# Six consecutive rows of a head per partition for q and k

## The reference

```python
q_d = q.reshape(B, H, Sd, 4, D).mean(axis=3)      # and k_d, v_d: groups of four positions
out_up = np.repeat(sm_attn(q_d, k_d, v_d), 4, axis=2)
mask = np.abs(pos[:, None] - pos[None, :]) < 4    # local window
scores = np.where(mask, scale * (q @ k.T), -1e9)
out = out_up + softmax(scores) @ v
```

## Time and profile before

| | |
|---|---|
| three runs | 876.13, 876.4, 880.44 us, median 876.4 |
| span of the profiled execution | 876.4 us |
| TensorE busy | 825.6 us (94%) |
| VectorE, ScalarE, GpSimd busy | 509.4, 406.7, 332.7 us |
| q and k copies out of PSUM | 16 on ScalarE for qT, 5 on ScalarE and 11 on VectorE for kT |
| DMA | 85.49 MB in 99,301 packets, 63,664 of them under 512 B |

### The profile page before, as it was taken

How to read it: one execution, slowest core, us unless ns; L and a number is a source line. 1 busy time by engine, 2 the same in 40 slices (tenths; PEclk the granted TensorE clock), 3 DMA queues, 4 the chain that set the end, 5 groups by cost and what they waited for, 6 DMA issues and landing times. The chain is left out here.

```text
span 876.4 us, 21162 instructions
## 1 busy us (share of the span) xinstructions
PE 825.6 (94%) x7658; PEld 747.9 (85%) x7658; DVE 509.4 (58%) x1424; ACT 406.7 (46%) x1006; POOL 332.7 (38%) x391
## 2 busy tenths in 40 slices
PE   6979999999999999999999999939999999999995
PEld 4867888888888888888998989838999999999995
DVE  4668766655755665563434344376766766756620
ACT  4655555444534444553444444304455454454461
POOL 6661133203311331240000000007776786787782
PEclk9899999999999999999999999958999999999998
DMA  9975521321322223201101000005624625615511
GB/s 199 255 194 136 142 67 42 94 80 27 79 79 63 57 79 79 66 1 39 50 1 48 0 24 2 24 21 201 220 95 163 231 64 187 227 46 217 204 53 45
DMA packets 99301, 85.49 MB, mean 98 GB/s; under 512 B 63664, under 2 KB 71856, under 8 KB 99248
## 3 DMA queue, kind: packets, MB, share of 16 engines
q1 hardware_dynamic: 93808, 74.74, 29.7%
q0 software_dynamic: 3072, 9.44, 3.7%
q10 hardware_dynamic: 2368, 0.59, 0.4%
HBM read 70.60 MB, written 14.16 MB: 97 GB/s over the span
## 5 line engine op out<-in xcount | busy, mean ns | idle before, releaser
L528 PE MATMUL PS<-xs,W 128*128 128x256 f32 x1728 | 234.1, 285 | 1.3 <-DVE xT L432 1.3
L528 PEld LDWEIGHTS PS<-xs,W 128*128 128x128 f32 x1728 | 222.6, 189 | 12.4 <-issue 3.3
L528 PE MATMUL PS<-W,g 128*128 128x512 f32 x864 | 223.9, 396 | 5.3 <-DVE g L669 5.0
L528 PEld LDWEIGHTS PS<-W,g 128*128 128x128 f32 x864 | 152.5, 188 | 37.4 <-DVE g L669 9.7
L633 ACT ACTIVATE scratch<-PS,minus 128x256 f32<-128x256 f32 x144 | 68.1, 473 | 218.7 <-DVE scratch L660 218.7
L660 DVE TENSOR_SCALAR scratch<-PS 128x256 f32<-128x256 f32 x144 | 61.0, 423 | 124.4 <-PE PS L528 123.9
L441 POOL TENSOR_TENSOR P<-P,top 128x640 f32<-128x640 f32 x11 | 13.9, 1261 | 224.8 <-DVE top L391 224.8
L1539 POOL TENSOR_TENSOR w1s<-w1r,w1s 128x512 fp32r<-128x512 f32 x64 | 80.7, 1287 | 28.2 <-ACT w1s L1427 27.9
L1334 PE MATMUL PS<-exs,w1s 128*128 128x288 f32 x256 | 81.1, 317 | 0.0
L1334 PE MATMUL PS<-ehs,w2s 128*128 128x288 f32 x256 | 80.8, 316 | 0.0
L1335 PE MATMUL PS<-exs,w1s 128*128 128x288 f32 x256 | 76.0, 297 | 0.0
(11 more groups left out here) (198 smaller groups left out, 1433.3 us busy)
## 6 DMA issues: line engine op xcount, KB each, us to landing
w1r<-in_moe_w SPq DMA_DIRECT2D x16, 1024.0 KB, 5.1
w2r<-in_moe_w SPq DMA_DIRECT2D x16, 1024.0 KB
vd<-in_v SPq DMA_DIRECT2D x16, 288.0 KB
xt<-xT SPq DMA_DIRECT2D x16, 288.0 KB, 2.2
y<-scratch SPq DMA_DIRECT2D x18, 256.0 KB, 2.2
vw<-in_v SPq DMA_DIRECT2D x34, 128.0 KB, 2.8
scratch<-in_moe_w_in SPq DMA_DIRECT2D x8, 512.0 KB, 5.9
scratch<-in_moe_w_out SPq DMA_DIRECT2D x8, 512.0 KB, 4.8
```

The lines of the kernel that those rows point to most:

```text
L528: r = pe.matmul(psum, wsel(w[i]), xsel(x[j]), start=first and t == 0, stop=last and t == 2)
```

## The change

The loads of q and k take the rows in another order: partition p now gets the six consecutive rows 6 p to 6 p + 5 of a head, so the transposed block j holds the positions 6 p + j. The copies from PSUM put them back in order: they read PSUM as before and write with a step of six elements along p, block j of bank b beginning at element 3 b + j. Everything behind the copies reads the same `qT` and `kT`. The pad columns of `qT`, the number of instructions, the waits and the order stay.

```diff
--- before.py
+++ after.py
@@ -204,13 +204,13 @@
             odd = odd_early(n)
             for h in heads:
                 eng.dma_start((qn_odd if odd else qn)[:, :, h, :],
-                              qf[ds(2 * n + h, 1), :, :].rearrange("h (j p) d -> p (h j) d", j=TJ)).then_inc(q_odd_loaded if odd else q_loaded, 16)
+                              qf[ds(2 * n + h, 1), :, :].rearrange("h (p j) d -> p (h j) d", j=TJ)).then_inc(q_odd_loaded if odd else q_loaded, 16)
 
         def load_k(eng, n, heads=(0, 1)):
             odd = odd_early(n)
             for h in heads:
                 eng.dma_start((kn_odd if odd else kn)[:, :, h, :],
-                              kf[ds(2 * n + h, 1), :, :].rearrange("h (j p) d -> p (h j) d", j=TJ)).then_inc(k_odd_loaded if odd else k_loaded, 16)
+                              kf[ds(2 * n + h, 1), :, :].rearrange("h (p j) d -> p (h j) d", j=TJ)).then_inc(k_odd_loaded if odd else k_loaded, 16)
 
         def load_vd(sp, n):
             sp.dma_start(vd[:, :, :, :, :].rearrange("p h i j d -> p h (i j d)"),
@@ -328,13 +328,21 @@
 
             return PS[:, T:T + 2, 0:cols]
 
+        def turned(T):
+
+            return both(T, S // 2).rearrange("m b (j p) -> m b j p", p=TP)
+
+        def in_order(x):
+
+            return x.rearrange("m (p b j) -> m b j p", b=2, j=JB)
+
         def act_qT(act, n, T):
             act.wait_ge(heads_turned, 2 * n + 1)
-            act.activation(qT[:, 0:S].rearrange("m (b t) -> m b t", b=2), both(T, S // 2), ACT.Copy).then_inc(qT_ready, 1)
+            act.activation(in_order(qT[:, 0:S]), turned(T), ACT.Copy).then_inc(qT_ready, 1)
 
         def act_kT(act, n, T):
             act.wait_ge(heads_turned, 2 * n + 2)
-            act.activation(kT[:, :].rearrange("m (b t) -> m b t", b=2), both(T + 2, S // 2), ACT.Copy).then_inc(kT_ready, 1)
+            act.activation(in_order(kT[:, :]), turned(T + 2), ACT.Copy).then_inc(kT_ready, 1)
 
         def act_exp(act, n):
             act.wait_ge(centred, n + 1)
@@ -369,7 +377,7 @@
 
         def dve_kT(dve, n, T):
             dve.wait_ge(heads_turned, 2 * n + 2)
-            dve.tensor_copy(kT[:, :].rearrange("m (b t) -> m b t", b=2), both(T + 2, S // 2)).then_inc(kT_ready, 1)
+            dve.tensor_copy(in_order(kT[:, :]), turned(T + 2)).then_inc(kT_ready, 1)
 
         def dve_pool_k(dve, n):
```

## The result

The changed kernel takes 883.46 us (median of 6 runs, 882.67 to 885.78). The kernel before, timed beside it, takes 877.1 us (6 runs, 875.68 to 880.44). The ratio is 1.0062, with a 95% interval of 1.0041 to 1.0083: slower by 0.6%, where no change was forecast, and above the range too (its upper end was 882.7). The profiled execution has a span of 881.9 us against 876.4, so +5.5 us.

What follows compares the result with a forecast made beforehand. TensorE, busy nearly throughout 64 to 380 us, was taken as the bound, with idle time in an opening where DMA runs behind. Forecast: 876.4 + 0 (loads) + 0 (copies) = 876.4 us; range 873.5 to 882.7 us.

Steps and rivals of the forecast that it cites:

- Where to look: From 64 to 380 us the change acts only where TensorE waits today; in the opening, on a chain through all engines.
- mixed stage: Dense layer interleaved with attention, 64 to 380 us; forecast 0, or 3.7 to 4.4 us added if strided writes cost more.
- the five at step 1: TensorE's waits for g behind VectorE's kT copy at 134, 195, 255, 316, 376 us; any addition counts in full.
- rival 1: Copies of qT and kT: 24 B write step takes two engine steps or more; slower, 880.1 to 882.7 us; chance 0.33.
- step-9 turns: Second unit turn in each chunk from the second on; 0.86 us of cover, enough for 0.61 or 0.73 us added.
- The copies at 0: Copies of qT and kT from PSUM: writing with a 24 B step adds 0 us, as the engine's own pace decides.
- the rival: The slower case for the qT and kT copies: + 0.48 us each on ScalarE, + 0.61 on VectorE; chance 0.33.
- The opening: First five head pairs, 5 to 56 us: costlier copies would add 0 to 1.9 us, nearer 0.
- The wait for v: TensorE's wait of 1.97 us at 50.47 us, unit 4; claimed able to swallow all of the opening's 1.9 us.
- The loads at 0: Loads of q and k: still 576 packets of 256 B per head, no change of DMA time, 0 us.
- Rival 2: Loads of q and k: larger packets or better-placed reads gain 1.2 to 2.9 us, 873.5 to 875.2 us; chance 0.12.
- The wait for v of unit 3: GpSimd's wait of 2.37 us in the opening; was to show whether the DMA backlog moved.

Runs made afterwards that it cites:

- e5_act_only: Changed kernel with only ScalarE's copies writing at the 24 B step; VectorE's kT copy reads PSUM with a step and writes densely: ratio 1.0013 (0.9993 to 1.0034).
- e3_psum_step: Changed kernel with all three copies permuting on the read: PSUM read with a step, SBUF written without one: ratio 1.0011 (0.9995 to 1.0028).
- m1_steps: Not the kernel: 128x576 copies alone at various read and write steps; f32 from PSUM, ScalarE 651 ns dense, 1172 strided; VectorE 758 and 1158.
- c1_before: The kernel before, unchanged, profiled a second time to see how far single profiles wander; 1.8 us earlier at 617 us than its first profile.
- e1_copies: Changed kernel with q and k loaded in the old order and the new strided copies kept (output order wrong): ratio 1.0039 (1.0025 to 1.0052).
- whole_six: Not the kernel: single head loads in the new order into a tile with a head's rows side by side, 1536 B pieces on both sides: issue 328 ns.
- c2_after: The changed kernel, unchanged, profiled a second time; from the first chunk to 400 us it lost 5.0 us where 3.6 were expected.
- e6_dve_only: Changed kernel with only VectorE's kT copy (units 5 to 15) writing at the 24 B step; ScalarE's copies write densely: ratio 1.0048 (1.0031 to 1.0065).

## Why the prediction was wrong, point by point

- **Where to look** was right. The mixed stage felt the change only through TensorE's waits, at the places named: the five at step 1 grew from 0.40 to 0.91 us (rival 1 had said 1.0), and the step-9 turns, with their 0.86 us of cover, stayed covered. The sixth, 77.94 us, grew by 0.51 us; its size goes with the clock ahead of it (it is 0.80 us in a third profile of the changed kernel, c3_after, with a clock of 0.79 from 64 to 72 us). "The qT copy on ScalarE starts before the kT copy does" is false there: e5_act_only shows that ScalarE's copy would hold up the same place by itself. One place was missed, a wait of 0.39 us at 114.45 us, behind the turn of unit 6, that the kernel before didn't have.
- **The copies at 0** was the step that failed: the write with a step of 24 B costs 0.60 us per copy on ScalarE and 0.525 us on VectorE. "ScalarE's pace is the same from PSUM and from SBUF" is a statement about reads, and so is every row; none has a write with a step. e3_psum_step and m1_steps show that reads from PSUM are free at any step tried and that the write alone pays. The text called this its weakest step and gave the rival 0.33; the rule of 16 B lines (the Trainium skill, page "Advanced Engine Details and Errata", SBUF Cachelines), the one statement at hand that bears on writes with a step, should have outweighed an argument from reads.
- **The rival's sizes.** + 0.48 us on ScalarE measured 0.60, + 0.61 on VectorE measured 0.525: not a doubling of each engine's pace but one common pace of the write. Six places at 0.61 us gave 3.7 us; the six that were there at 0.51 to 0.53 us and the new one of 0.39 make 3.5 of the 3.6 us measured from the first chunk to 400 us.
- **The opening**, "0 to 1.9 us, nearer 0", gave 1.95. The wait for v was to swallow the 1.9 us of units 2 and 3. But unit 4's own two copies stand ahead of the same wait and were not in the sum: its copy of qT starts 3.20 us late (49.32 us for 46.12), its copy of kT ends 4.25 us late (51.56 for 47.31), TensorE takes up its scores 3.97 us late (51.66 for 47.69), and the wait of 1.97 us gives back only its own length. It isn't always as long, either: 0.78 us in c1_before. The loads' delay adds to this, but a loss of this kind doesn't need it: with the old loads e1_copies, in its one profile, still lost 1.58 us.
- **The range** was missed by 0.8 us, and that by its base. The rival's 880.1 to 882.7 us, taken as spans, hold the profiled 881.9. But in every run on record the time is 1.7 to 1.8 us above the span of the same execution (883.67 and 881.9 here), so the profiled span of 876.4 us belongs to an execution of about 878.2 us. That it equalled the median of the runs, 876.4, was chance, and "nothing is added" was wrong. With 1.8 us added the rival's times are 881.9 to 884.5 us and hold the measured 883.46.
- **The loads at 0.** Packets were right: 2368 on ScalarE's queue in both, one for each row of 256 B and the closing ones. That a loss by the loads "has a lead of a whole unit to eat first" failed for unit 0, which has none: its queue time per load went from 0.41 to 0.74 us and k came 0.9 us late. Rival 2, a gain of 1.2 to 2.9 us, had the wrong sign; whole_six shows that even whole pieces land only 0.2 us sooner. The wait for v of unit 3, named as the sign of a shorter backlog, did vanish in the first profile (and is 2.38 us in c2_after), and meant the opposite: everything ahead of it was late, not the landing early.

## What to carry to other kernels

Ask of every copy that permutes which side takes the step. From PSUM the read took every step tried without cost, while neighbours 16 B or more apart in SBUF make a write of f32 go at 2.0 ns per element on either engine; so permute on the read. Then price the edit where an engine's queue ends in a wait of TensorE: here VectorE's 0.525 us counted six times in full, and ScalarE's 0.60 us, outside the opening, at one or two places of chunk 0 only. Where copies of several units stand ahead of one wait, count them all before setting the wait against them. Contiguous rows in DRAM bring nothing if the tile in SBUF breaks them up, and the first load of a kernel has no lead, so that a longer issue can show in full. And before a sum of spans is called a time, compare a run's time with the span of that same run.

## What the runs showed of the hardware that was not expected

- The two engines, 651 and 758 ns when dense, come to the same 1158 to 1172 ns when writing 24 B apart from PSUM. From SBUF to SBUF VectorE does the same in 676 ns (460 dense).
- ScalarE pays for reading SBUF at a step as for writing it (1202 and 1215 ns at six elements, 682 dense), but nothing for reading PSUM at a step (651 ns).
- bf16 writes at a step are dearer than f32 ones of the same distance (ScalarE, from PSUM): 2080 ns at 12 B, 2691 ns at 24 B, where f32 took 928 and 1172 ns.
- The time that a load occupies its queue depends on how its two sides are cut: 313 ns when the source has runs of 256 B, 570 ns when it has longer ones and the destination is cut into 256 B, 328 ns when both are whole, for the same bytes.
- The same stretch of the same program is granted different clocks in different executions: from 64 to 72 us the changed kernel had 1.00, 0.60 and 0.79 of full speed in three profiles, and 0.57 in e6_dve_only. Differences of 1 to 2 us between single spans go with this, as much as the parts of the change that were to be told apart.
